# Value products of a banded attention turned round: one column half of TensorE's array per head

## The reference, cut to what matters

```python
# q, k, v: (2, 8, 768, 64); n_sink = 4, window = 128
scores = scale * np.matmul(q, k.transpose(0, 1, 3, 2))
keep = is_sink | in_window                       # per query: 128 keys before it, and 4 sinks
scores = np.where(keep, scores, -1000000000.0)
scores = scores - np.max(scores, axis=-1, keepdims=True)
a = np.exp(scores)
a = a / (np.sum(a, axis=-1, keepdims=True) + 1e-09)
x = np.matmul(a, v)                              # -> tokens (1536, 512)
# mixture of experts: skip where x @ w_skip <= 0, else argmax of x @ w_gate picks one of 8
y[mask] = gate_w[mask, None] * (np.maximum(xc[mask] @ w1[e], 0.0) @ w2[e])
# dense layer: (1536, 512) @ (512, 2048), ELU, @ (2048, 512)
```

## Time and profile before

| | before |
|---|---|
| median of 3 runs | 553.14 us (551.63 to 553.38) |
| the profiled execution: its time, and its span | 552.9 us, 551.1 us |
| busy: PE, PEld | 537.2 us (97%), 463.2 us (84%) |
| busy: DVE, ACT, POOL | 271.8 us (49%), 216.2 us (39%), 50.5 us (9%) |
| granted clock of TensorE | 1.000 over the span |

### The profile page before, as it was taken

How to read it: one execution, slowest core, us unless ns; L and a number is a source line. 1 busy time by engine, 2 the same in 40 slices (tenths; PEclk the granted TensorE clock), 3 DMA queues, 4 the chain that set the end, 5 groups by cost and what they waited for, 6 DMA issues and landing times.

```text
span 551.1 us, 9074 instructions
## 1 busy us (share of the span) xinstructions
PE 537.2 (97%) x3312; PEld 463.2 (84%) x3313; DVE 271.8 (49%) x726; ACT 216.2 (39%) x429; POOL 50.5 (9%) x108
## 2 busy tenths in 40 slices
PE   8999999999899999999999999999999999999997
PEld 4777777777489999999989999999999999999996
DVE  7566655554795245446766634333343333433332
ACT  4565655554044244445644423322233222332222
POOL 6000000000111101111120000400004000020000
PEclk9999999999999999999999999999999999999999
DMA  9478787342119659999952000300003000010001
GB/s 194 128 255 300 264 297 260 109 138 77 50 36 346 225 192 348 368 349 352 359 167 77 0 1 0 103 13 1 2 0 114 0 0 0 1 58 0 1 0 59
DMA packets 46957, 72.24 MB, mean 131 GB/s; under 512 B 16452, under 2 KB 16708, under 8 KB 46916
## 3 DMA queue, kind: packets, MB, share of 16 engines
q1 hardware_dynamic: 42018, 61.35, 33.2%
q0 software_dynamic: 2400, 7.87, 4.5%
q10 hardware_dynamic: 2498, 2.51, 1.3%
HBM read 57.56 MB, written 14.16 MB: 130 GB/s over the span
## 4 chain that ended last, share of the span: by engine, by line
PE 94%; DVE 3%; issue 1%; ACT 1%; ACTq 0%; POOL 0%; DVEq 0%; POOLq 0%
PE ps_out L1715 24%; PE ps_g L1379 24%; PE ps_h L1640 12%; PE ps_y L1379 9%; PE ps_pv L1477 7%; PE ps_qk L1400 6%; PE ps_turn L1431 4%; PE ps_turn L1459 2%; PE ps_pv L1489 1%; DVE prob L1045 1%; PE ps_turn L1447 1%; PE ps_x L1582 1%; PE ps_x L1678 1%; PE ps_turn L1439 1%; PE ps_pv L1405 1%
## 5 line engine op out<-in xcount | busy, mean ns | idle before, releaser
L1379 PE MATMUL ps_g<-x_hi,w_hi 128*128 128x384 f32 x252 | 85.1, 338 | 0.0
L1379 PE MATMUL ps_g<-x_lo,w_hi 128*128 128x384 f32 x252 | 84.7, 336 | 0.0
L1379 PE MATMUL ps_g<-x_hi,w_lo 128*128 128x384 f32 x252 | 84.6, 336 | 0.0
L1353 DVE TENSOR_SCALAR g_raw<-g_raw 128x384 f32<-128x384 f32 x64 | 23.1, 361 | 117.4 <-ACT g_raw L956 117.4
L956 ACT ACTIVATE g_raw<-ps_g 128x384 f32<-128x384 f32 x64 | 31.5, 492 | 125.7 <-PE ps_g L1379 123.0
L1715 PE MATMUL ps_out<-w_hi,g_hi 128*128 128x512 f32 x192 | 75.4, 393 | 0.2
L1715 PE MATMUL ps_out<-w_hi,g_lo 128*128 128x512 f32 x192 | 75.5, 393 | 0.0
L1715 PE MATMUL ps_out<-w_lo,g_hi 128*128 128x512 f32 x192 | 75.3, 392 | 0.0
L1640 PEld LDWEIGHTS ps_h<-xg_t,up_w 128*128 128x128 f32 x576 | 65.6, 192 | 1.6 <-ACT xg_t L899 0.9
L1640 PE MATMUL ps_h<-xg_t,up_w 128*128 128x128 f32 x576 | 65.9, 275 | 0.7 <-ACT xg_t L899 0.7
L960 ACT ACTIVATE g_hi<-g_raw 128x384 fp32r<-128x384 f32 x64 | 33.7, 526 | 62.2 <-DVE g_raw L1356 62.2
(11 more groups left out here) (196 smaller groups left out, 721.2 us busy)
## 6 DMA issues: line engine op xcount, KB each, us to landing
raw<-in_moe_w SPq DMA_DIRECT2D x16, 1024.0 KB, 6.4
up_w<-in_moe_w SPq DMA_DIRECT2D x16, 1024.0 KB, 10.5
raw<-in_moe_w_in SPq DMA_DIRECT2D x4, 1024.0 KB, 6.4
raw<-in_moe_w_out SPq DMA_DIRECT2D x4, 1024.0 KB, 6.8
rows<-zeros SPq DMA_DIRECT2D x2, 1792.0 KB, 9.6
v_pad<-in_v SPq DMA_DIRECT2D x16, 192.0 KB, 5.1
rows<-x_tok SPq DMA_DIRECT2D x6, 512.0 KB, 4.5
k_pair<-in_k SPq DMA_DIRECT2D x7, 432.0 KB, 4.6
```

The lines of the kernel that those rows point to most:

```text
L1353: dve.tensor_scalar(g_raw[f % GB][:], g_raw[f % GB][:], 1.0, 1.0, ALU.min, ALU.subtract).then_inc(g_min_done, 1)
L1379: last = pe.matmul(to, w, x, start=start and m == 0, stop=stop and m == 2)
```

## The change

Seven things are changed together.

1. **Value products turned round.** In `pv` the values are now the weights (64 columns, one head), and the turned probabilities move (128 columns). Head h uses the columns h*64 to h*64 + 63 of the array (`tile_position`) and writes the same partitions of PSUM. The result stands with the head's dimensions on partitions and queries along the row. The two heads alternate. The values are loaded as they are: `v_pair` takes the place of `v_pad`, its memsets and its ones go.
2. **Sums.** `exponentials` have an accumulator output, `sums`, and VectorE's `invert(g)` works from it.
3. **The turn back.** ScalarE copies the group's values out of PSUM undivided (`xt_sb`); TensorE turns them back into the same bank and multiplies them with `wg_heads` (the routing weights with the other head's rows zero, 18 columns per unit).
4. **Division behind the turn.** VectorE's `normalise(g)` scales both results by `invs`: `gate_heads`, then `x_tok`. `add_gates(g)` adds the two heads' parts and adds them to `scores`.
5. **Order.** In an even step: `turn_sinks` and `turn_unit(u)`, `turn_x`, `qk(u + 2)`, `pv(u - 1)`; in an odd one: `turn_unit(u)`, `sinks_pv`, `qk(u + 2)`, `pv(u - 1)`. The turned sinks lie beside the unit's tiles and one copy takes both. `turn_unit` waits for `turned_a` and `turned_b` alone. There are 51 steps, not 52.
6. **Routing.** The 12 comparisons become three instructions, for 6, 4 and 2 tiles (`HERE`), both times; one addition to `slot` goes into the reduction before it.
7. **First gather.** VectorE writes the first chunk's tokens straight to `source_i`; GpSimd's copy and its `idle` instruction ahead of the first gather go.

```diff
@@ scalar: exponentials @@
-                    act.activation(out_, out_, ACT.Exp, bias=low[:, n % 4:n % 4 + 1],
-                                   scale=-1.0).then_inc(prob_ready, 1)
+                    act.activation(out_, out_, ACT.Exp, bias=low[:, n % 4:n % 4 + 1], scale=-1.0,
+                                   accum_out=sums[u // 2 % 4][:, n % 4, :]).then_inc(prob_ready, 1)
@@ vector: behind the turn back @@
+                def normalise(g):
+                    t, c = place_of(g)
+                    by_head = invs[g % 2][:].rearrange("p (t h) o -> p t h o", h=2)
+                    dve.wait_ge(inv_ready, 2 * g + 2)
+                    dve.wait_ge(x_turned, g + 1)
+                    dve.tensor_tensor(gate_heads[g % 2][:],
+                                      ps_pv[g % 2][:, 2 * P:2 * P + 2 * GE].rearrange("p (t h e) -> p t h e", t=2, h=2),
+                                      by_head.broadcast_to([P, 2, 2, E1]), ALU.mult).then_inc(gate_scaled, 1)
+                    dve.tensor_tensor(x_tok[:, t:t + 2, c * P:(c + 1) * P].rearrange("p t (h d) -> p t h d", h=2),
+                                      ps_pv[g % 2][:, 0:2 * P].rearrange("p (t h d) -> p t h d", t=2, h=2),
+                                      by_head.broadcast_to([P, 2, 2, DH]), ALU.mult).then_inc(normalised, 1)
@@ tensor @@
-                    if x_turned_at(u - 1) is not None:
-                        pe.wait_ge(xt_kept, x_turned_at(u - 1) + 1)
-                    if gate_at(u - 1) is not None:
-                        pe.wait_ge(gate_added, gate_at(u - 1) + 1)
+                    g = sinks_beside(u)
+                    if g is not None:
+                        turn_sinks(g, len(key_tiles(u % QT)))
...
-                    for h in range(2):
-                        for m, (tile, _) in enumerate(key_tiles(i)):
-                            last = pe.matmul(ps_pv[g % 2][:, u % 2 * PV:(u % 2 + 1) * PV], prob_t[u % 2][:, h, m, :],
-                                             v_pad[p % 2][h][:, tile, :], start=(u % 2 == 0 and h == 0 and m == 0),
-                                             stop=(i == 1 and h == 1 and m == 1), skip_group_check=True)
+                    for m, (tile, _) in enumerate(tiles):
+                        for h in range(2):
+                            cols = slice(h * DH, (h + 1) * DH)
+                            last = pe.matmul(ps_pv[g % 2][cols, u % 2 * P:(u % 2 + 1) * P], v_pair[p % 2][:, tile, cols],
+                                             prob_t[u % 2][:, h, m, :], start=(u % 2 == 0 and m == 0),
+                                             stop=(i == 1 and m == 1), skip_group_check=True, tile_position=(0, h * DH))
@@ routing, both times @@
-            for t in range(NT):
-                dve.tensor_scalar(here[:, t, :], lane[:, 0, :], slot[:, t, :], None, ALU.is_equal).then_inc(here_ready, 1)
+            for lo, hi in zip(HERE, HERE[1:]):
+                dve.tensor_tensor(here[:, lo:hi, :], lane[:].broadcast_to([P, hi - lo, P]),
+                                  slot[:, lo:hi, :].broadcast_to([P, hi - lo, P]), ALU.is_equal).then_inc(here_ready, 1)
```

More of the change, by code:

```diff
@@ L43, in build @@
     SLOTS_W = NP2
+    HERE = (0, 6, 10, 12)
     RAW = 3
@@ L213, in build @@
                 invs = [sb(f"invs{i}", [P, 4, 1]) for i in range(2)]
-                prob_t = [sb(f"prob_t{i}", [P, 2, 2, P]) for i in range(2)]
+                prob_t = [sb(f"prob_t{i}", [P, 2, 3, P]) for i in range(2)]
                 sink_p = sb("sink_p", [P, 4, SK])
-                sink_t = sb("sink_t", [P, P])
+                sums = [sb(f"sums{i}", [P, 4, 1]) for i in range(4)]
+                gate_heads = [sb(f"gate_heads{i}", [P, 2, 2, E1]) for i in range(2)]
+                gate_sum = [sb(f"gate_sum{i}", [P, 2, E1]) for i in range(2)]
                 xt_sb = sb("xt_sb", [P, 2, P])
@@ new lines, in add_gates @@
+                def add_gates(g):
+                    t, c = place_of(g)
+                    heads = [gate_heads[g % 2][:, :, h, :] for h in range(2)]
+                    dve.wait_ge(gate_scaled, g + 1)
+                    if c == 0:
+                        dve.tensor_tensor(scores[:, t:t + 2, :], heads[0], heads[1], ALU.add).then_inc(gate_added, 1)
+                    else:
+                        n = g - (g // (PC * PG) + 1) * PG
+                        dve.tensor_tensor(gate_sum[g % 2][:], heads[0], heads[1], ALU.add).then_inc(gate_joined, 1)
+                        dve.wait_ge(gate_joined, n + 1)
+                        dve.wait_ge(gate_added, g - PG + 1)
+                        dve.tensor_tensor(scores[:, t:t + 2, :], scores[:, t:t + 2, :], gate_sum[g % 2][:],
+                                          ALU.add).then_inc(gate_added, 1)
@@ L1085, in _ @@
                                         ps_turn[1][:, 0:tiles, :]).then_inc(turned_b, 1)
[L1086 to L1092 removed]
+                    g = turned_beside(u)
+                    if g is not None:
+                        normalise(g)
                     if u < 2:
```

238 lines of the change are left out of this document (98 added, 140 removed).

## The result

The changed kernel takes 531.19 us (median of 6 runs, 530.20 to 532.29), the kernel before 552.45 us on the same chip (6 runs, 551.63 to 553.38): ratio 0.9616, 95% interval 0.9601 to 0.9632. The gain is 21.3 us where 12.5 were said (the forecast counted from 553.14). The direction and the main mechanism are right; what was taken for the rest of a pair's time, and for the routing, was not.

The account below looks back on a forecast made before the run. TensorE's work per pair of heads was taken to bound the attention, VectorE the routing. Attention -13.9, tail +0.3 and routing +1.1 summed to -12.5 us: 540.6 us from 553.14, range 533 to 551.

Parts of the forecast that it names:

- Rival A: Whole kernel: column halves run side by side, shape changes cost what they do now; 540.6 us, 535 to 545, chance 0.66.
- (4): Attention, TensorE's turn: the wait for `gate_added`, VectorE's scores, goes; -0.35 us per pair of heads.
- (3): Attention: first weight load behind `qk` becomes always that of 64-column values, 0.08 us each; +0.21 us per pair.
- (8): Routing: larger comparison pieces delay TensorE, whose own time the loop is; +0.44 and +0.66, together +1.1 us.
- (1): Attention, value products: column halves run at the same time, 22 passes count for 44; -2.51 us per pair.
- (2): Attention: one more change of array shape per step, gap 0.09 and load 0.05; +0.84 us per pair.
- (5): Attention: sinks, turns, turn back and scores need the same passes as before; nothing gained or lost.
- (6): Attention, ScalarE and VectorE: extra work from sums, `gate_heads` and additions fits in their room; nothing on the path.
- (7): Tail, from the attention's steps to the last scores: 5.2 us for 4.93, +0.3 us.
- B: Attention: another engine or a latency sets the pace, above all where quarters are split; 547 us, chance 0.16.
- C: Value products: the column halves take turns; 559 us, slower by 1%, chance 0.11.
- D: Value products: halves run side by side but their weight loads are no longer hidden; 550 us, chance 0.04.

Follow-up runs that it names:

- e8: The changed kernel with the scores of both units of a pair computed in the even step, none in the odd one: 528.40 us, ratio 0.9564.
- e9: e8 with both units' value products also in the even step and the group's turn back in the next odd step: 532.14 us, ratio 0.9626.
- e2: The kernel before, with VectorE adding the routing scores ahead of its second mask and `x_tok`: 550.98 us, ratio 0.9966.
- e7: The changed kernel without the exponentials' accumulator output, a constant 128 in place of the sums: 530.42 us, ratio 0.9600.
- e1: The changed kernel with value products back on the whole array, values padded with zeros to 128 columns: 546.62 us, ratio 0.9888.
- e4: The changed kernel with twelve filling products for seven ahead of the routing's first count product: 530.64 us, ratio 0.9597.
- e6: The changed kernel with each unit's value products issued one head after the other, not alternating: 531.59 us, ratio 0.9615.
- e5: The changed kernel with the turn back and the scores' products (even steps) moved behind `qk`, one more array shape change there: 536.00 us, ratio 0.9701.

## Why the prediction had the mechanism right and the time wrong

The time, 531.19 us, lies below the range: it falls in the forecast's rest ("better than 535"), which had a chance of 0.03. Rival A's mechanism came true, its sum did not. Three steps of it failed: the wait of (4) was taken from one row's idle time, the loads of (3) from one group's length, and the routing's loop in (8) was put down to TensorE.

**Per pair of heads: forecast -1.81, measured -2.76.** Times 7.67 that is 7.3 us more than forecast, the largest part of the 9.1 by which the profiled executions beat the forecast's gain (21.6 for 12.5).

- (1) Passes side by side: right, to the size. Forecast -2.51. In e8 and the changed kernel eight passes, gap and load included, take 0.59 us; e9 has sixteen in 1.02 (17.18 to 18.20), so eight more cost 0.44, 0.109 for each two. 22 times that is 2.40, for 4.93.
- (2) The third shape: right. Forecast +0.84, six times a gap of 0.09 and a turn's load of 0.05. The gap is 0.09 to 0.10, and four turns behind column halves take 0.49 for 0.44.
- (3) The loads behind `qk`: forecast +0.21, measured about -0.15. I read the four gate products behind `qk` (0.47) as holding 0.02 of load. The kernel before has the same four products between other work of the whole array, in its tail, in 0.37:

```profile
135.22 0.51 PE L1459 MATMUL ps_turn<-wg,xt_sb 128*128 128x9 f32 x4
135.59 1.14 PE L1477 MATMUL ps_pv<-v_pad,prob_t 128*128 128x130 f32 x8
```

So 0.10 of load had stood there three times a pair all along, and the change took it away; and the load of 64 columns that came in its place is about 0.06, not 0.08. This reading of a group's length against passes that weren't timed alone is the first step that failed. (2) and (3) together: forecast +1.05, measured about +0.70, a miss of 0.35. (A change of shape isn't all that lays such a load open: behind the bf16 fills of the tail the four take 0.46, too, 137.87 to 138.33.)

- (4) The wait: forecast -0.35, what the profile puts down to VectorE's scores. Start to start it was 0.52 (91.57 to 92.54, less 0.45), because the row's duration runs over the end of streaming. With it went the wait in front of the turned sinks behind the narrow `qk` (0.59 us to the next start before, 0.42 now) and two small ones (eight value passes took 0.96 and not 0.89 at 82.82 and at 86.15): together about -0.8. **This is the step that was mis-sized most, by 0.45.** e2 shows that this gain isn't that of the one wait either: with the scores early, 0.22 came.
- (5) "Nothing" for sinks, turns, turn back and scores: the turn back is 0.22 for 0.25 three times, -0.10, and some -0.05 more elsewhere.
- (6) VectorE and ScalarE: right that they are not on the path. No wait for them shows in a plain pair and e7 leaves it at 13.29. The exponentials' sums cost ScalarE 0.19 each, within the bounds of 0.08 and 0.20; its 9.25 us of a pair lie below the 10 to 11 of the sum. Where quarters are split one pair takes 0.25 us more.

Sum of the measured terms: -2.51 + 0.70 - 0.8 - 0.15 = -2.76; the terms marked "about" are read from single rows, and the -0.05 is what was left over. e1 cuts the sum once more in two, without these readings: -1.88 with the halves and -0.88 without, where the forecast's terms give -1.46 and -0.35. So both parts were forecast too small.

**(7) The tail**: forecast +0.3, measured -0.05. **The start** of the 46 steps, which I left alone, came 0.78 earlier: the turn of step 1 started at 9.83 and not 10.43, with 0.43 us idle before it and not 0.82, and the four value passes behind took 0.37 for 0.55. **(8) The routing**: forecast +1.1, measured +0.10 from the last scores on. The step "it is TensorE's own time" was wrong: at the same clock of 1.00 24 products and their fills take 1.47 us, so the 2.47 before was VectorE's twelve pieces (2.44) with TensorE behind them, and I had given this the weaker weight. With it the larger pieces cost nothing, where +0.44 and +0.66 were forecast. What they and the shorter way to the first reduction (0.26 us from the scores to `top`, for 0.65) gave, the clock took back: 0.90 us, by e4. The forecast had such a pause in its rest and not in its sum. The 1.0 us of this miss, 0.35 and 0.78 are the rest of the 9.1, to 0.3.

**The rivals.** B is small: one pair with quarters takes 0.25 us more than a plain one, a wait ahead of the turned sinks, and the sums aren't its cause (e7); a plain pair has none. C fell with e6 and with 0.59 us for eight passes. D: the weight loads of the column halves are 136 ns each, 44 in a pair, and hidden, for two of them and two passes go by in 0.109 us:

```profile
L1460 PEld LDWEIGHTS ps_pv<-prob_t,v_pair x44: 132/136/137, 70.4 to 81.7; 128*64 128x64 f32 x44
```

The Trainium skill (TensorE: Matmul & The Clock Gate, Part 3) would have them exposed, since both halves share their rows; this trace disagrees. On the change of shape, the Trainium skill (TensorEngine Tiling, Key Properties) says that it drains the engine. The trace agrees, with a gap of 0.09 to 0.10 us each time.

## What to carry to other kernels

Two float32 products of 64 output columns run side by side in column halves, in both orders of issue that were tried; what eats into the factor of two is the change of array shape, 0.15 to 0.20 us each time by what is loaded first behind it, so blocks of one shape belong together, up to the point where the copies between them lose their cover. Price a removed wait from start to start, not by the idle time in brackets, and look for the second wait behind it: taken alone it gave 0.22 us a pair, where its place had lost 0.52. And price a load or a gap by the same instructions in two surroundings, never by one group's length.

## What the hardware showed that I had not expected

- A change of shape costs about the same between two split shapes as between a split one and the whole array: the wide `qk` takes 0.68 us to the next start with column halves behind it (72.03 to 72.71) and 0.69 with a turn on the whole array (87.45 to 88.14 before). It is 0.09 to 0.10 us until the next start, and 0.05 or 0.06 (a turn, 64-column values) to 0.11 us (float32 weights of 128 columns) of load. e5's extra one took 0.15 without its wait, those that e8 takes away 0.20 each.
- An exponential with a sum is two instructions on ScalarE: 527 ns and a read of the accumulator of 187 ns.
- The granted clock fell to 0.50 for 6.8 us in the routing of the changed kernel, behind 1.43 us without work and thin products, and to a mean of 0.63 over 4 us behind a wait of 1.43 us for keys in e8. With the pause in the routing filled (e4) it stayed at 1.00 there, and once (e7) it stayed there with the pause as well.
